# A code shift ahead of TensorE's level loop, and a new order of three copies in the opening of a fused attention and MLP kernel

## The reference

```python
# 1: decayed linear attention, B=4, H=8, S=768, D=48
for t in range(S):
    state = alpha[:, :, t, :, None] * state + einsum('bhd,bhe->bhde', k[:, :, t], v[:, :, t])
    y[:, :, t] = einsum('bhd,bhde->bhe', q[:, :, t], state)
# 2: rank-32 token mixing and an MLP 384 -> 1536 -> 384
u = x + (xt @ U @ V).transpose(0, 2, 1)
x = u + maximum(u @ w_ch1, 0) @ w_ch2
# 3: gated MLP with a 768 x 768 spatial product
h = maximum(x @ w_in, 0); u, v = split(h)
out = (u * (einsum('ts,bsd->btd', w_spatial, norm(v)) + b)) @ w_out
```

## Time and profile before

| what | value |
|---|---|
| median of 3 runs | 728.79 us (727.12 to 729.78) |
| profiled execution, its own time | 727.21 us |
| its span from first to last instruction | 725.0 us |
| granted TensorE clock, mean share of full | 0.988 |
| busy: PE, PEld, DVE, ACT, POOL | 696.3, 660.6, 392.6, 340.2, 212.0 us |
| DMA moved | 49.48 MB |
| instruction queue (q8) | 77 packets, 1.26 MB |
| batch 0's keys for group 0 landed | 9.13 us |

### The profile page before, as it was taken

How to read it: one execution, slowest core, us unless ns; L and a number is a source line. 1 busy time by engine, 2 the same in 40 slices (tenths; PEclk the granted TensorE clock), 3 DMA queues, 4 the chain that set the end, 5 groups by cost and what they waited for, 6 DMA issues and landing times.

```text
span 725.0 us, 25711 instructions
## 1 busy us (share of the span) xinstructions
PE 696.3 (96%) x11336; PEld 660.6 (91%) x11336; DVE 392.6 (54%) x666; ACT 340.2 (47%) x575; POOL 212.0 (29%) x143
## 2 busy tenths in 40 slices
PE   2689999999999999999999999999999999999998
PEld 2688989899899999999999999999998998999998
DVE  6888665545654654655453415125834852871671
ACT  5887654554654454556444332335532432532422
POOL 6704660410450320351220330461360060043022
PEclk9879999999999999999999999999999999999999
DMA  9415410410401221401100341011110101101001
GB/s 360 169 47 168 163 42 8 154 47 10 149 3 46 80 79 46 156 3 47 37 3 3 101 151 66 33 38 62 65 45 23 66 23 43 65 0 65 0 0 65
DMA packets 16524, 49.48 MB, mean 68 GB/s; under 512 B 1616, under 2 KB 9552, under 8 KB 15920
## 3 DMA queue, kind: packets, MB, share of 16 engines
q1 hardware_dynamic: 16432, 48.09, 18.8%
HBM read 38.65 MB, written 9.44 MB: 66 GB/s over the span
## 4 chain that ended last, share of the span: by engine, by line
PE 92%; ACT 3%; DVE 2%; issue 1%; DMA 1%; SPq 0%; DVEq 0%; ACTq 0%
PE HB L906 25%; PE ZB L994 7%; PE ZB L996 7%; PE ZB L995 7%; PE SB L906 6%; PE SB L782 5%; PE SB L1031 5%; PE ZB L906 4%; PE SB L888 2%; PE SB L1035 2%; PE ZB L1031 2%; PE ZB L1044 2%; PE SB L897 2%; PE SB L843 2%; PE SB L1044 2%
## 5 line engine op out<-in xcount | busy, mean ns | idle before, releaser
L1556 DVE SCALAR_TENSOR_TENSOR hid_lo<-HB,hid_hi 128x384 fp32r<-128x384 f32 x92 | 51.2, 556 | 139.7 <-ACT hid_hi L1238 139.3
L1238 ACT ACTIVATE hid_hi<-HB 128x384 fp32r<-128x384 f32 x92 | 45.3, 492 | 158.6 <-PE HB L906 158.5
L994 PE MATMUL ZB<-hid_hi,w2h 128*128 128x384 f32 x288 | 98.2, 341 | 0.0
L906 PE MATMUL HB<-uh,w1h 128*128 128x384 f32 x276 | 97.8, 354 | 0.2 <-DVE ul L1552 0.2
L996 PE MATMUL ZB<-hid_lo,w2h 128*128 128x384 f32 x288 | 96.5, 335 | 0.0
L995 PE MATMUL ZB<-hid_hi,w2l 128*128 128x384 f32 x288 | 96.3, 334 | 0.0
L906 PE MATMUL HB<-ul,w1h 128*128 128x384 f32 x276 | 92.5, 335 | 0.0
L906 PE MATMUL HB<-uh,w1l 128*128 128x384 f32 x276 | 92.4, 335 | 0.1
L1085 ACT COPY Qd<-Q 48x768 f32<-48x768 f32 x84 | 73.1, 871 | 12.8 <-POOL Q L674 4.3
L731 POOL TENSOR_TENSOR gl<-gf,gh 128x384 fp32r<-128x384 f32 x32 | 33.5, 1048 | 144.1 <-ACT gh L1278 143.8
L674 POOL TENSOR_TENSOR Q<-Q,bk 112x768 f32<-112x768 f32 x14 | 25.6, 1827 | 162.7 <-ACT Qd L1085 162.7
(11 more groups left out here) (269 smaller groups left out, 1516.5 us busy)
## 6 DMA issues: line engine op xcount, KB each, us to landing
Q<-in_q SPq DMA_DIRECT2D x8, 768.0 KB, 6.1
AL<-in_al SPq DMA_DIRECT2D x7, 768.0 KB, 4.5
K<-in_k SPq DMA_DIRECT2D x7, 768.0 KB, 4.2
Vt<-in_v SPq DMA_DIRECT2D x8, 576.0 KB, 3.6
mid<-x2s SPq DMA_DIRECT2D x8, 576.0 KB, 3.7
x<-mid SPq DMA_DIRECT2D x4, 1152.0 KB, 5.4
out<-o_sb SPq DMA_DIRECT2D x24, 192.0 KB, 1.8
x2s<-in_w SPq DMA_DIRECT2D x9, 384.0 KB, 5.1
```

The source lines that it names most:

```text
L906: last = nc.tensor.matmul(dst, weights(x, w), moving(y, m), start=(n == 0 and x == y == 0), stop=(n == total - 1 and y == 1))
L994: nc.tensor.matmul(bank, w2h[:, i, cols], hi, start=(i == 0), stop=False)
L1238: nc.scalar.activation(hid_hi[:, i % HID, :], up_bank(i)[:, 0:TILE], ACT.Relu).then_inc(h_hi, 1)
L1556: nc.vector.scalar_tensor_tensor(hid_lo[:, i % HID, :], up_bank(i)[:, 0:TILE], 0.0, hid_hi[:, i % HID, :].bitcast(F32), ALU.max, ALU.subtr ...
```

## The change

Four edits. PE increments the semaphore `passed`, for which nobody waits, 64 times before its first wait and the level loop. ACT walks over the opening's steps in another order: group 1's transposed keys (`T_STEP`) before group 1's level 7 score copies, with the first weight casts tied to the step that is now last of the two; the third set of group 1's transposes goes to the bank ZB[0] instead of ZB[2]. On DVE the square copies of both groups, which stood between the level 6 and level 7 scalings, are parted: group 0's after its level 7 key scaling, group 1's after `key_copies` of group 0.

```diff
+SHIFT = 64
...
-HIGH1 = {(1, T_STEP): [0, 1], (0, KV_STEP): [2, 3], (0, Y_STEP - 1): [4], (1, Y_STEP - 1): [5]}
+HIGH1 = {(1, LEVELS - 1): [0, 1], (0, KV_STEP): [2, 3], (0, Y_STEP - 1): [4], (1, Y_STEP - 1): [5]}
...
+ACT_LAST = [(0, MASKED), (1, MASKED), (0, LEVELS - 1), (1, T_STEP), (1, LEVELS - 1)]
...
-        side_space.SB, side_space.TB, side_space.KVB, side_space.YB = ZB, HB + ZB[2:], HB[1], ZB
+        side_space.SB, side_space.TB, side_space.KVB, side_space.YB = ZB, HB + ZB[:1], HB[1], ZB
...
+            for _ in range(SHIFT):
+                pe.sem_inc(passed, 1)
             pe.wait_ge(zeroed_s, 4)
             with pe.Fori(0, MASKED) as n:
...
-            for g, n in LAST_STEPS:
+            for g, n in ACT_LAST + [s for s in LAST_STEPS if s not in ACT_LAST]:
                 if n == MASKED:
                     square_copies(0, g, QUARTERS[:2])
                 att_step(0, g, n, True)
...
-                if (g, n) == (1, MASKED):
-                    for h in range(GROUPS):
-                        square_copies(h, QUARTERS[2:])
+                if (g, n) == (0, LEVELS - 1):
+                    square_copies(0, QUARTERS[2:])
                 if (g, n) == (0, T_STEP):
                     key_copies(g)
+                    square_copies(1, QUARTERS[2:])
```

## The result

The changed kernel takes 736.50 us (median of 6 runs, 734.40 to 739.09) against 727.34 us (6 runs, 726.41 to 729.78): a ratio of 1.0121, 95% interval 1.0095 to 1.0148, so slower by 9 us. The forecast was 730.1 us, range 725.6 to 732.4. The profiled execution has a span of 734.1 us against 725.0. Ratios compare means of fast runs: they leave out the few executions that took over 1.5% more than the fastest of their kernel (two of twelve in "Queries first", one of twelve in "All together").

The account below looks back on a forecast made before the run. PE, busy 96% of the span, was taken as the bound. A first-pass stop of +3.3 us less a 2.0 us gain gave +1.3 us on the 728.79 us median: 730.1 us, range 725.6 to 732.4.

Parts of the forecast that it names:

- What bounds the kernel: Opening step: PE is busy 96% of the span, so an opening gain or loss moves the rest equally.
- First-pass stop: In the level loop's first pass PE stands 3.6 us for the third code block, delaying ACT's spread: +3.3 us.
- the fetch comes in time: Rival: the third block's fetch starts before about 14 us, leaving only the gain, 725.9 to 727.7 us; chance 0.16.
- The increments: 64 increments before PE's first wait, 0.10 us each, fit in idle time: nothing to 0.3 us, taken as nothing.
- The level 6 hole: PE's 1.83 us stop in the second group's level 6 goes: gain 1.07 us, 2.9 if the clock stays up.
- the middle of 2.0: Gain taken for removing the level 6 stop, 2.0 us, between 1.07 and 2.9 us if the clock stays up.
- The reordering: New copy orders on DVE and ACT around the opening's transposes cost nothing and protect the 1.07 us gain.
- The gain carried on: Later stretches are full of matmuls, so the opening's gain moves the rest of the kernel by the same amount.
- The loop over three blocks: Rival: the level loop's three code blocks are fetched anew each pass, some 16 us, 744 us; chance 0.05.
- Turns between queues: DMA engines alternating queues by packet would remove the first-pass stop; the 18 to 19 us fetch was read against it.

Follow-up runs that it names:

- Queries first: Old kernel with batch 1's first-group queries issued ahead of the three weight pieces; 730.53 us, ratio 1.0019.
- All together: Old kernel plus copy orders, 16 tiny matmuls before the loop, 40 before the first group's level 7, queries ahead of weight pieces; 731.37 us, ratio 1.0057.
- Increments only: Old kernel with only the 64 increments in front of the loop, old copy order; 736.05 us, ratio 1.0117.
- the late pad: Old kernel with 16 tiny matmuls (64 instructions) added only at the start of the first token mixing, near 61 us; 736.40 us, ratio 1.0121.
- the shift by 224: Old kernel with 56 tiny matmuls (224 instructions) in front of the loop, nothing else; 728.72 us, ratio 1.0006.
- the loads left out: Changed kernel without the loads of queries, values and decays for batch 1's second group; 729.67 us, ratio 1.0024 to the old kernel.
- the cheap shift: Changed kernel with 16 tiny matmuls (64 instructions) in front of the loop instead of the increments; 735.11 us, ratio 1.0100 to the old kernel.

## Why the prediction was wrong

The step that failed is in "What bounds the kernel": later stretches are full of matmuls, "so a gain or loss in the opening moves the rest of the kernel by the same amount". I followed the moved code only to the end of the level loop. All unrolled code behind it moves too, and each block end with it. Increments only, the late pad alone and the shift by 224 show that the loss of 9 us comes from there and not from the opening. The fetches near 78 us are late in both kernels: the block entered at 73.84 us before has its successor fetched at 78.02, the one entered at 74.20 us after the change at 78.18. What the shift moved is the place where the block runs out: at about 80.1 us among long matmuls before, at 78.81 us inside a burst of short ones after, so that PE stood 1.72 us. The run with the loads left out shows that this fetch is late because of the data. As the trace reads, the second stop follows from the first: PE's program, out of its lead, met its own wait 0.4 us after the block's entry, and the fetch came behind the wait and the data (7.5 us in all). Then PE's half clock and, in the late pad's trace, slow key scalings of DVE add to it. The old trace had the material: a hole of 0.25 us at 80.39 shows that the block end there came only just behind its fetch. Of the forecast's terms:

- *First-pass stop, +3.3 us: did not happen.* The prediction took the one fetch in 18 to 19 us as the delay under load. It came at 15.2 us after the change, at 13.6 with the cheap shift, and with the loop at its old place at about 14.0, 14.0, 18.1 and 18.9 us in four traces. One row was one draw from a range of 5 us. The first pass wanted its block near 17.8 us, since the loop itself began 1.65 us later. The rival "the fetch comes in time" had the outcome right, but it asked for a start before 14 us: 15.2 and the 2.4 us behind it make 17.6, in time by luck of the increments' own delay.
- *The increments, 0 us: they cost 1.65.* PE's first level began at 11.11 instead of 9.46 us. In the trace they are 0.15 us apart, 9.8 us in all, where I had taken 0.10 from control instructions at the loop's head. The prediction's bound of 0.3 us was too low.
- *The level 6 hole, -1.07 us or more: right.* The hole is gone, with a wait of 1.24 us for DVE's query scaling in its place (0.76 was said, and 1.2 for the whole stand). From the first level to token mixing PE won 2.4 us on the old kernel (1.65 late at the start, 0.77 ahead at 60.81), so the middle of 2.0 was fair; the clock was at half only from 41.0 to 44.4 us.
- *The reordering: right, and alone worth nothing* (1.0016). The transposes did meet ACT for 0.4 us, which was not foreseen.
- *The gain carried on: wrong too.* By 68.75 us PE was 0.26 us behind the old kernel, since the queries were issued at 60.02 instead of 59.45 us, behind weight pieces (from 57.96 us, before from 57.31) that wait for DVE's splits.
- *The loop over three blocks* did not refetch. Between 16 and 36 us the changed kernel's trace has a single instruction fetch, near 27 us, while the loop made five more passes. The two lines that the page "Runtime: NRT & Kernel Launch" of the Trainium skill names ("Instruction fetch mechanics") do not hold for this loop; the 128 KiB that the same section gives for PE would.
- *Turns between queues.* Of the 7.5 us behind 80.53, 4.5 lie before the end of PE's own wait and the quiet fetches' 1.0 us comes on top, which leaves about 2 us for the data (an estimate from these rows); the fetch of 78.18 us was late by about 2.7 us against the run without the loads. The page "DMA: Bandwidth & Descriptors" ("Queues, rings and completion order"), also of the Trainium skill, has turns by packet. Whether such turns allow 2 to 3 us no run shows, and the prediction's single row at 18 us could not decide it either.

Open: why a wait of PE's program holds a fetch back in some cases while other fetches start inside a wait, and what decides how long a fetch stands behind data. The traces show when a fetch ran, not when it was asked for, and which DMA engine served it isn't known. Whether the late block in the first pass ever stalls the changed kernel can't be told either; no trace showed it.

## What to carry to other kernels

Code placement is global: whoever pads one spot of an unrolled program moves every block end behind it, so look at all stretches where short instructions run in bursts, beside heavy loads or right behind a wait, not at the spot alone. A hole labelled "issue" inside a row of like instructions, with one instruction fetch that starts 2.2 to 2.5 us ahead of its end, is the mark; an "issue" ahead of a whole row can be a plain wait, so look at what ended just then. And a delay read from a single DMA packet under load is one draw: give it the width of the range before it enters a sum.

## What the runs showed that I had not expected

A semaphore increment on PE cost 0.15 us. A tiny matmul, which moves the code by four instructions, took 0.07 to 0.12 us (48 in 3.22 us, 16 in 1.91 us): 64 places cost 9.8 us by increments and 1.9 us by tiny matmuls, and padding by matmuls in front of the loop started level 0 at 9.45 us, by increments at 11.11. This is cheap but not free: 48 of them in the opening took over 4 us. And a block's fetch started from under 1 to 7.5 us after the block before it was entered, behind data or behind PE's own wait, enough to turn a move of 64 instructions into 1.2% of the kernel.
